# First chunk of a three-stage kernel: queries, scores, masks and values handed on in halves, second queries on VectorE, constants issued by ScalarE's queue

## The reference, cut to what matters

```python
def _attn_ref(q, k, v):                      # (4, 8, 768, 64)
    gamma = 1.0 - 2.0 ** (-5.0 - np.arange(H, dtype=np.float32))
    scale = 1.0 / np.sqrt(D)
    for t in range(S):
        state = gamma[None, :, None, None] * state + np.einsum('bhd,bhe->bhde', k[:, :, t], v[:, :, t])
        y[:, :, t] = scale * np.einsum('bhd,bhde->bhe', q[:, :, t], state)

def _moe_ref(x, w_in, w_out, alpha):         # (3072, 512), 512 -> 2048 -> 512
    h = x @ w_in
    g = np.maximum(h, 0.0) + alpha * np.minimum(h, 0.0)
    return g @ w_out
```

## Time and profile before

| | |
|---|---|
| median of 3 runs | 948.07 us |
| lowest, highest | 947.96, 949.17 us |
| profiled execution, its own time | 947.68 us |
| its span in the trace | 945.6 us |
| granted TensorE clock, mean | 0.997 of full speed |
| TensorE busy | 934.3 us, 99% |
| VectorE busy | 667.5 us, 71% |
| ScalarE busy | 314.9 us, 33% |
| GpSimd busy | 261.1 us, 28% |

### The profile page before, as it was taken

How to read it: one execution, slowest core, us unless ns; L and a number is a source line. 1 busy time by engine, 2 the same in 40 slices (tenths; PEclk the granted TensorE clock), 3 DMA queues, 4 the chain that set the end, 5 groups by cost and what they waited for, 6 DMA issues and landing times.

```text
span 945.6 us, 15972 instructions
## 1 busy us (share of the span) xinstructions
PE 934.3 (99%) x5537; PEld 788.1 (83%) x5537; DVE 667.5 (71%) x1180; ACT 314.9 (33%) x436; POOL 261.1 (28%) x193
## 2 busy tenths in 40 slices
PE   8999999999999999999999999999999999999996
PEld 7888888888888888888888888889988889888885
DVE  4555579747984698558965897786786667799641
ACT  4232121112111121112111221245566666678541
POOL 4443215331434134422433232512021111100101
PEclk9999999999999999999999999999999999999998
DMA  8432297024001500140002302168856668799611
GB/s 291 161 131 79 82 386 258 1 90 146 0 0 45 189 0 0 39 149 24 1 8 94 123 1 90 46 231 308 302 200 243 227 230 299 288 358 380 226 43 55
DMA packets 32898, 137.64 MB, mean 146 GB/s; under 512 B 5280, under 2 KB 5792, under 8 KB 24114
## 3 DMA queue, kind: packets, MB, share of 16 engines
q1 hardware_dynamic: 25186, 118.27, 34.8%
q0 software_dynamic: 4480, 12.74, 3.5%
q10 hardware_dynamic: 3168, 5.79, 1.8%
HBM read 124.16 MB, written 26.31 MB: 159 GB/s over the span
## 4 chain that ended last, share of the span: by engine, by line
PE 98%; DMA 1%; DVE 0%; SPq 0%; issue 0%; POOL 0%; POOLq 0%; ACT 0%
PE bank L796 28%; PE bank L814 28%; PE bank L958 16%; PE bank L889 6%; PE bank L927 5%; PE bank L922 3%; PE bank L682 2%; PE bank L726 2%; PE bank L698 2%; PE bank L781 1%; PE bank L924 1%; PE bank L715 1%; PE bank L937 1%; DMA attention<-in_qk 1%; PE bank L921 0%; DVE en_all L1058 0%
## 5 line engine op out<-in xcount | busy, mean ns | idle before, releaser
L796 PE MATMUL bank<-activations_split,weights_split 128*128 128x512 f32 x1152 | 277.7, 391 | 0.0
L814 PE MATMUL bank<-weights_split,activations_split 128*128 128x512 f32 x1152 | 276.3, 389 | 0.0
L814 PEld LDWEIGHTS bank<-weights_split,activations_split 128*128 128x128 f32 x1152 | 216.1, 188 | 45.2 <-POOL activations_split L1899 0.4
L796 PEld LDWEIGHTS bank<-activations_split,weights_split 128*128 128x128 f32 x1152 | 215.1, 188 | 45.9 <-issue 1.1
L1899 POOL TENSOR_TENSOR activations_split<-scratch,activations_split 128x512 fp32r<-128x512 f32 x84 | 123.6, 1472 | 301.8 <-ACT activations_split L1630 297.0
L1630 ACT CAST activations_split<-scratch 128x512 fp32r<-128x512 f32 x96 | 59.8, 622 | 409.8 <-DVE scratch L1101 409.8
L958 PE MATMUL bank<-weights_split,activations_split 128*128 128x512 f32 (+1 forms) x648 | 158.1, 395 | 0.0
L958 PEld LDWEIGHTS bank<-weights_split,activations_split 128*128 128x128 f32 x648 | 118.8, 188 | 23.3
L1096 DVE TENSOR_SCALAR scratch<-bank,alpha 128x512 f32<-128x512 f32 x96 | 71.7, 747 | 91.8 <-PE bank L796 90.8
L1329 DVE TENSOR_TENSOR weights_split<-attention,weights_split 128x2048 fp32r<-128x2048 f32 (+1 forms) x45 | 102.2, 2286 | 18.8 <-ACT weights_split L1710 18.6
L1958 POOL DMA_INDIRECT out<-scratch,y_token x27 | 38.6, 1429 | 261.3 <-ACT scratch L1743 260.7
(11 more groups left out here) (271 smaller groups left out, 865.7 us busy)
## 6 DMA issues: line engine op xcount, KB each, us to landing
attention<-in_w_exp SPq DMA_DIRECT2D x48, 1024.0 KB, 6.5
en_all<-in_w_exp SPq DMA_DIRECT2D x16, 1024.0 KB, 7.0
attention<-in_kv SPq DMA_DIRECT2D x43, 256.0 KB, 4.2
expert_rows<-in_pad_rows SPq DMA_DIRECT2D x8, 1285.0 KB, 25.4
rows<-in_w_mlp SPq DMA_DIRECT2D x14, 512.0 KB, 3.9
attention<-in_qk SPq DMA_DIRECT2D x12, 512.0 KB, 5.6
rows<-expert_rows ACTq DMA_DIRECT2D x22, 257.0 KB, 4.6
scratch<-in_qk SPq DMA_DIRECT2D x10, 512.0 KB, 3.6
```

What stands on the lines that cost most here:

```text
L796: last = mm(H_ps[f % 2][:, :], win(a, kc, f), x[:, kc, :], start=(k == 0), stop=(k == 3 * KC - 1))
L814: last = mm(bank[j][:, :], x[f % 2][:, j * P:(j + 1) * P], wout(a, f), start=(f == 0 and a == 0 and part_ == "hi"), stop=(f == FB - 1 and ...
```

## The change

It has five parts, all in the first chunk and ahead of it:

1. Scores, masks and values of a head pair are split in two parts of two batches. `A_first[part][head]` is now bank 4 + 2 part + head: both sets of banks serve every head pair, part 0 in banks 4 and 5, part 1 in 6 and 7. `first_scores` and `first_mixed_values` issue part 0 and part 1 one behind the other, each with its own wait (`s_q_part`, `s_q_pool`, `s_m_part`, and `s_m` for the second part); `first_masked` issues four operations of 256 columns in place of two of 512.
2. Head pair 1's queries are scaled by VectorE (`first_query(1)`), behind the masks of head pair 0; GpSimd keeps head pairs 2 and 3. All first queries are scaled in two parts.
3. The two first loads of constants are issued by ScalarE's queue, ahead of its table load, in place of SyncE's.
4. Values 3 are loaded before weight block 0, and ScalarE scales them before it splits that block. VectorE's residual of head pair 0 moves behind the masks of head pair 2.
5. `first_hidden` takes, for each of 4 input blocks, the high product and the residual product, waiting for each input apart (`s_xh`, `s_xl`), and the four low-weight products last; the wait for the low half of the weights stands ahead of those.

```diff
-    A_first = [[A_ps[:, 0], A_ps[:, 1]], [b3(6), b3(7)]]
+    HB = B // 2
+    A_first = [[bank[4 + 2 * k + hh][:, 0:HB * P].rearrange("p (b c) -> p b c", b=HB) for hh in range(2)] for k in range(2)]
...
-            sp.dma_start(C[:, :QD + P], consts[:, :QD + P]).then_inc(s_masks, 16)
             load_qk(0, 0)
             load_v(0, 0)
-            sp.dma_start(C[:, QD + P:MASKS], consts[:, QD + P:MASKS]).then_inc(s_masks_rest, 16)
             load_qk(0, 1)
...
             load_v(0, 2)
+            load_v(0, 3)
             load_w(0)
-            load_v(0, 3)
             load_w(1)
...
+            def first_scores(hp):
+                for part_ in range(2):
+                    if hp < 2:
+                        pe.wait_ge(s_q_part, due(s_q_part, 2 * hp + part_ + 1))
+                    else:
+                        pe.wait_ge(s_q_pool, due(s_q_pool, 2 * (hp - 2) + part_ + 1))
+                    if hp and part_ == 0:
+                        pe.wait_ge(s_m_part, due(s_m_part, hp))
+                    elif hp:
+                        pe.wait_ge(s_m, due(s_m, hp))
+                    for b in range(HB * part_, HB * (part_ + 1)):
...
+                    last.then_inc(s_A_part if part_ == 0 else s_A, 1)
+
+            def first_mixed_values(hp):
+                scaled(0, hp)
+                for part_ in range(2):
+                    if part_ == 0:
+                        pe.wait_ge(s_m_part, due(s_m_part, hp + 1))
+                    else:
+                        pe.wait_ge(s_m, due(s_m, hp + 1))
...
+            def first_hidden(f):
+                pe.wait_ge(s_whi, due(s_whi, f + 1))
+                pe.wait_ge(s_g, due(s_g, 0 if f < 2 else f - 1))
+                for kc in range(KC):
+                    if f == 0:
+                        pe.wait_ge(s_xh, due(s_xh, kc + 1))
+                    mm(H_ps[f % 2][:, :], win(0, kc, f), x_hi[:, kc, :], start=(kc == 0), stop=False)
+                    if f == 0:
+                        pe.wait_ge(s_xl, due(s_xl, kc + 1))
+                    mm(H_ps[f % 2][:, :], win(0, kc, f), x_lo[:, kc, :], start=False, stop=False)
+                low_done(pe, f)
+                for kc in range(KC):
+                    last = mm(H_ps[f % 2][:, :], win(1, kc, f), x_hi[:, kc, :], start=False, stop=(kc == KC - 1))
+                last.then_inc(s_h, 1)
...
+            def first_query(hp):
+                if hp:
+                    dve.wait_ge(s_masks_rest, due(s_masks_rest, 16))
+                dve.wait_ge(s_qk_ld[hp], due(s_qk_ld[hp], 16))
+                for part_ in range(2):
+                    some = qT(0, hp)[:, HB * part_:HB * (part_ + 1), :]
+                    ve.tensor_tensor(some, some, qdecay[:, hp:hp + 1, :].broadcast_to([P, HB, P]), ALU.mult)\
+                      .then_inc(s_q_part, 1)
+
+            def first_masked(hp):
+                if hp >= 2:
+                    dve.wait_ge(s_Y, due(s_Y, hp - 1))
+                for part_ in range(2):
+                    if part_ == 0:
+                        dve.wait_ge(s_A_part, due(s_A_part, hp + 1))
+                    else:
+                        dve.wait_ge(s_A, due(s_A, hp + 1))
+                    for hh in range(2):
...
             def first_attention():
-                for hp in range(HP):
...
+                first_query(0)
+                first_masked(0)
+                first_query(1)
+                first_masked(1)
+                first_masked(2)
+                x_low(0, 0)
+                first_masked(3)
                 for hp in range(1, HP):
                     x_low(0, hp)
                 split_w(1)
...
+            se.dma_start(C[:, :QD + P], consts[:, :QD + P]).then_inc(s_masks, 16)
+            se.dma_start(C[:, QD + P:MASKS], consts[:, QD + P:MASKS]).then_inc(s_masks_rest, 16)
             act.wait_ge(s_zero, due(s_zero, 1))
...
             first_values(2)
+            first_values(3)
             split_w(0)
             x_high(0, 1)
-            first_values(3)
...
-            for hp in range(1, HP):
-                query_decay(0, hp)
+            for hp in range(2, HP):
+                pool.wait_ge(s_qk_ld[hp], due(s_qk_ld[hp], 16))
+                for part_ in range(2):
+                    some = qT(0, hp)[:, HB * part_:HB * (part_ + 1), :]
+                    gp.tensor_tensor(some, some, qdecay[:, hp:hp + 1, :].broadcast_to([P, HB, P]), ALU.mult)\
+                      .then_inc(s_q_pool, 1)
```

More of the change, by code:

```diff
@@ L359, in build @@
     s_qk_ld = [sem(f"qk_ld{i}") for i in range(HP)]
[L360 removed]
+    s_vs_first, s_wlo_pool, s_zero, s_tau, s_masks_rest = sem("vs_first"), sem("wlo_pool"), sem("zero"), sem("tau"), sem("masks_rest")
+    s_q_part, s_q_pool, s_A_part, s_m_part = sem("q_part"), sem("q_pool"), sem("A_part"), sem("m_part")
     s_k_ld = [sem(f"k_ld{i}") for i in range(2)]
@@ L684, in scores @@
                 last.then_inc(s_A, 1)
+            def first_scores(hp):
[10 more added lines that the diff above has]
+                        for hh in range(2):
+                            rows = slice(hh * D, (hh + 1) * D)
+                            last = mm(A_first[part_][hh][:, b % HB, :], kT(0, hp)[rows, b, :], qT(0, hp)[rows, b, :],
+                                      start=True, stop=True)
+                    last.then_inc(s_A_part if part_ == 0 else s_A, 1)
[6 more added lines that the diff above has]
+                        pe.wait_ge(s_m, due(s_m, hp + 1))
+                    for b in range(HB * part_, HB * (part_ + 1)):
+                        for hh in range(2):
+                            cols = slice(hh * D, (hh + 1) * D)
+                            last = mm(Y_of(0, hp)[cols, b, :], v_sb(0, hp)[:, b, cols], mixed_of(0, hp)[:, hh, b, :],
+                                      start=True, stop=True)
+                last.then_inc(s_Y, 1)
             def from_state(c, hp):
@@ L716, in to_state, with values @@
                 last.then_inc(s_SU, 1)
-            def values(c, hp, first=False):
+            def values(c, hp):
                 u = 4 * c + hp
@@ L726, in values @@
                         last = mm(Y_of(c, hp)[cols, b, :], v_sb(c, hp)[:, b, cols], mixed[:, hh, b, :],
-                                  start=first, stop=(first or b == B - 1))
+                                  start=False, stop=(b == B - 1))
                 last.then_inc(s_Y, 1)
@@ L847, in _ @@
                 mm(bank[0][:, 0:P], idle_in, idle_in, start=True, stop=True)
-            scores(0, 0)
-            values(0, 0, first=True)
-            scores(0, 1)
+            first_scores(0)
+            first_mixed_values(0)
+            first_scores(1)
             for hp in range(1, HP):
                 if hp + 1 < HP:
-                    scores(0, hp + 1)
-                values(0, hp, first=True)
+                    first_scores(hp + 1)
+                first_mixed_values(hp)
             mlp(0)
```

32 lines of the change are left out of this document (11 added, 21 removed).

## The result

| | before | after |
|---|---|---|
| median of 4 runs | 948.07 us | 956.40 us |
| lowest, highest | 947.96, 949.17 us | 953.32, 956.62 us |
| profiled execution, its own time | 947.68 us | 956.62 us |
| its span | 945.6 us | 954.5 us |
| granted TensorE clock, mean | 0.997 | 0.995 |

The ratio after to before is 1.0078, with an interval of 1.0056 to 1.0099 (it goes by the means; between the medians lie 8.3 us). The kernel is slower by 7 to 8 us, where 946.7 and no measurable change were predicted. The time lies outside the whole range, 945.9 to 948.0.

What follows compares the result with a forecast made beforehand. TensorE (PE) bounds the kernel, so only its early idle, 2.8 us, could be saved. Handoffs, transfers and dense-layer start bring the first down product from 23.30 to 21.85: 1.45, taken as 1.4, giving 946.7 us; range 945.9 to 948.0.

Steps and rivals of the forecast that it cites:

- Later stretches pass it on: After the first down product: the 1.4 us gain survives, with 9.4 us of cover at ScalarE's next transfer wait.
- the slower one, starving constants: Rival at the start: constants on ScalarE's queue land late, delaying VectorE's first operation; up to 950.0 us, net loss chance 0.05.
- a wait that I do not see: Anywhere in the kernel: an unforeseen wait making it slower by over 0.2%, chance 0.02.
- 6.1 us is fixed: Kernel start: PE cannot begin scores before 6.1 us because the dummy matmuls are untouched.
- Halves: First chunk's attention handoffs: split masks take 1.43 us per head pair, 0.13 dearer, but let PE start parts earlier.
- The transfers: First loads: two issues leave SyncE's queue, so everything landing after 8 us lands 0.3 us earlier.
- The unused 0.48 us: DMA engines' idle share from 2 to 6 us, taken as all that could be filled; 0.3 of it counted.
- the end of 0.94: Upper end of the earlier landings, in us, if the issues rather than the DMA engines set the pace.
- the first rival: First loads: landings do not move at all; gain 1.05 us, down product 22.25, time 947.0 us, chance 0.25.
- The second rival: First loads: everything lands 0.7 us or more earlier; gain 1.95, down product 21.35, time 946.1 us, chance 0.2.
- The hidden group: First hidden group: PE starts at 16.15 and stops once, at the eighth pass, for the last residual, ready at 17.85.
- My last condition: Sign of being wrong: the first down product comes 1.4 us earlier and the total time does not.

Runs made afterwards that it cites:

- the one at offset 0: The changed kernel with a directive starting VectorE's middle-chunk loop at slot 0 to 2 of a 256-instruction block: 946.35 us, ratio to before 0.9973.
- offsets 12, 128 and 192: The changed kernel with the directive starting VectorE's loop at that slot of a 256-instruction block: 947.14, 951.24 and 953.78 us.
- the one with the old hidden order: The changed kernel with its loop at offset 0 and the first chunk's hidden products in the old order with the old waits: 947.54 us.

## Why the prediction was wrong

**The step that failed** is "Later stretches pass it on", with its reason that "PE's own chain has no other holder". I had followed data: what feeds each group of PE, and how much cover it has. I had not followed the instructions of an engine off the bound. VectorE is 71% busy and its loop had 1.65 us of wait at each turn, so it looked harmless. But the change puts 12 instructions ahead of that loop, and 12 empty instructions in the kernel before make the same loss. The sum should have held a term for every loop that a change shifts. From the trace of before it had no row: neither jump shows a wait but PE's 1.65. None of the rivals held it either; the slower one, starving constants, was the wrong mechanism, and only the chance of 0.02 for "a wait that I do not see" was left for what came. The clock, for which I counted nothing because the start ran at 1.00, held there and not behind the jumps: of the 10.3 us lost at them, 3.8 are not PE's waits but the time behind them at the lower clock.

In the terms of the profiled execution: -1.89 at the end of chunk 0 and -0.30 to the end of chunk 1, +5.52 and +4.76 at the jumps, +0.8 in the expert stage, which is the 8.9 us between the spans. The last 0.8 I did not settle. From chunk 5's landmark to the span's end the kernel before takes 333.2 us, the changed one 334.1, the one at offset 0 333.3, the one with 8 empty instructions 335.9, and those at offsets 12, 128 and 192 take 335.3 to 335.6. The stage varies with places too, or between runs, and 0.8 lies within that.

Point by point, the start:

- **PE's first scores at 6.1: right for this run (6.01), wrong as a reason.** I wrote that "6.1 us is fixed" by the dummy matmuls. Their row takes 5.02 us here and 5.49 in the run at offset 0, and ends at 5.64 in the one with the old hidden order: the first scores lie between 5.65 and 6.48 over all the runs. The eight profiles with the whole change reach the down product between 21.22 and 22.23, mean 21.57; the eight with the old start between 22.78 and 23.30, mean 23.03. That is 1.46 between the means, where 1.45 was forecast for one pair. The agreement to 0.01 is luck: the terms below were off by more, and each group spreads over 0.5 to 1.0.
- **Halves: right.** Four masks take 1.42 (1.43 predicted), two halves of the queries 0.76, two on GpSimd 1.41 (1.4). Values 0 at 7.67 (7.55), scores 1 at 8.83 (8.9), values 1 at 11.80 (11.9).
- **The transfers: mis-sized, 0.3 against 0.74 (0.4 to 0.9 over the profiles).** The unused 0.48 us did not bound it, because the share is a mean and the rate went up too: 348 GB/s between 4 and 6 us where the kernel before had 275. The issues set the pace; the end of 0.94 was the nearer one. By the rule that issuing from several engines saves only the sequencer's time (the Trainium skill, "DMA: Bandwidth & Descriptors", section "Issuing engines are not separate DMA queues") I had let the landings stay in the first rival. Two issues are 0.94 us of a sequencer's time, and 0.74 of it reached the landings; the rule holds, and I had drawn the wrong sum from it. (That rival also carries its shift of 0.3 to the down product as 0.4, 22.25 for 22.15; nothing hangs on it.)
- **The second rival is what the start did in this profile.** What landed behind the issues did so 0.7 earlier; it gave the last residual at 17.35 (17.24) and the down product at 21.35 (21.39). Its 946.1 is near the 946.35 that the version at offset 0 measured. I had given it 0.2.
- **The constants: later, and harmless, as forecast.** They land 4.5 us after their issue where they took 2.2, and VectorE starts at 5.38 (5.2 for the first queries' landing). That is the bringing in with the first queries which the taking of turns between queues suggested.
- **The hidden group: no stop.** I had expected one at the eighth pass; the last residual is ready at 17.24 and that pass starts at 17.53, since what feeds the residual came earlier; the weight block's split starts at 13.44 and not at 14.25.

My last condition, that the down product comes 1.4 earlier and the time does not, is what happened.

## What to carry to other kernels

When a change adds or removes instructions ahead of a loop, compare its turns with the ones before it: a row at the loop's head that waits 3 to 6 us behind "issue", or behind an engine that had long been running, with packets on an instruction queue in the same stretch, was here a fetch and no dependency. 64 empty instructions, a directive for the loop's place or a hint on its jump each took 9 to 10 us back here. Measure the place that you get: 12 and 24 empty instructions in the kernel before made the loss, and the directive at offsets 128 and 192 had a stall of its own. Judge a change of a start by its landmarks in the trace first, and only then by the total, which can have its own cause elsewhere.

## What the runs showed of the hardware

- A jump back can cost 1.6 to 5.5 us of kernel time though it is on an engine that is not the bound. At a bad place VectorE stood 3.5 to 5.8 us at a jump, and PE waited 1.3 to 3.6 us for it.
- Behind such a wait the granted clock sometimes fell to 0.50, and the length of the wait alone did not decide it. It fell behind waits of 3.62 and 2.87 us (the changed kernel), 3.36 (offset 192), the second of two of 2.7 (12 empty instructions) and 2.10 (24, the second); it stayed at 1.00 behind 3.06 (offset 128), the first of the two of 2.7 and 1.32 (24, the first). Where it fell, the chunk lost 1.9 us more than the wait, 2.9 at offset 192.
- The instruction queue tells such a loop from a good one: 10 or 11 packets between 180 and 425 us in the three kernels with stalls at the jumps, none or one in the fifteen without.
- It hangs on few places: a shift of 4 or 8 instructions did nothing at the jumps, 12 and 24 lost two turns, 40 and 76 none. Why these, with a loop of 253 instructions, stays open; I did not try the places between.
- The same 132 KB took 2.2 us to land when issued first on one queue and 4.5 us when issued on a second at the same moment as 512 KB on the first.
